# Retention in products of 64 by 64 by 64, with two state updates a chunk

## The reference, cut to what matters

```python
# q, k, v: (2 batches, 8 heads, 768 positions, 64)
gamma = 1.0 - 2.0 ** (-5.0 - np.arange(H))
for t in range(S):
    state = gamma[None, :, None, None] * state + einsum('bhd,bhe->bhde', k[:, :, t], v[:, :, t])
    y[:, :, t] = scale * einsum('bhd,bhde->bhe', q[:, :, t], state)
# x = y as (1536 tokens, 512); first mixture, 8 experts, F = 1024
P = exp(x @ w_gate - max); 8 rounds of row and column normalisation
out += P[:, e:e+1] * (maximum(x @ w1[e], 0) @ w2[e])      # for each e
# second mixture: 4 experts, weights from domain_probs, same form
```

## Time and profile before

| what | us |
|---|---|
| median of 3 runs (1549.5 to 1549.5) | 1549.5 |
| the profiled execution | 1548.59 |
| its span, first to last instruction | 1546.8 |
| PE busy | 1538.3 |
| DVE busy | 882.2 |
| ACT busy | 441.6 |
| POOL busy | 55.0 |

### The profile page before, as it was taken

How to read it: one execution, slowest core, us unless ns; L and a number is a source line. 1 busy time by engine, 2 the same in 40 slices (tenths; PEclk the granted TensorE clock), 3 DMA queues, 4 the chain that set the end, 5 groups by cost and what they waited for, 6 DMA issues and landing times.

```text
span 1546.8 us, 21387 instructions
## 1 busy us (share of the span) xinstructions
PE 1538.3 (99%) x8312; PEld 1395.1 (90%) x8312; DVE 882.2 (57%) x1419; ACT 441.6 (29%) x840; POOL 55.0 (4%) x45
## 2 busy tenths in 40 slices
PE   8999999999999999999999999999999999999999
PEld 7889988998899889988998899889998999899988
DVE  8656855555546545555464455576555556455553
ACT  4422321322223213222232132243331223213311
POOL 6200000000000000000000000012000000000000
PEclk9999999999999999999999999999999999999999
DMA  9100101101001011010010110101101001011011
GB/s 347 57 28 28 55 1 55 42 14 55 26 29 54 0 54 39 16 54 24 30 54 0 54 40 16 55 1 56 55 1 55 28 28 54 0 54 55 1 43 67
DMA packets 34602, 66.62 MB, mean 43 GB/s; under 512 B 2032, under 2 KB 2672, under 8 KB 34544
## 3 DMA queue, kind: packets, MB, share of 16 engines
q1 hardware_dynamic: 34112, 65.63, 12.2%
q10 hardware_dynamic: 432, 0.18, 0.0%
HBM read 62.66 MB, written 3.15 MB: 43 GB/s over the span
## 4 chain that ended last, share of the span: by engine, by line
PE 98%; DVE 1%; DMA 1%; issue 0%; SPq 0%; DVEq 0%
PE banks L1151 17%; PE banks L1152 17%; PE banks L1150 17%; PE banks L1129 15%; PE banks L1133 15%; PE banks L1131 15%; PE banks L1007 1%; DMA qt_in<-in_q_t 0%; PE banks L1042 0%; PE banks L1093 0%; PE banks L1037 0%; DMA small<-in_c_small 0%; DVE scores L637 0%; PE banks L1026 0%; PE banks L1073 0%; PE banks L1075 0%
## 5 line engine op out<-in xcount | busy, mean ns | idle before, releaser
L1129 PE MATMUL banks<-x_hi,w_hi 128*128 128x384 f32 x1344 | 449.9, 335 | 1.4 <-DVE w_lo L665 1.3
L1133 PE MATMUL banks<-x_hi,w_lo 128*128 128x384 f32 x1344 | 449.5, 334 | 0.0
L1131 PE MATMUL banks<-x_lo,w_hi 128*128 128x384 f32 x1344 | 449.3, 334 | 0.0
L1152 PE MATMUL banks<-w_hi,h_lo 128*128 128x512 f32 x1148 | 447.6, 390 | 0.0
L1151 PE MATMUL banks<-w_lo,h_hi 128*128 128x512 f32 x1148 | 447.4, 390 | 0.0
L1150 PE MATMUL banks<-w_hi,h_hi 128*128 128x512 f32 x1148 | 446.9, 389 | 0.0
L866 DVE SCALAR_TENSOR_TENSOR acc<-banks,gate,acc 128x512 f32<-128x512 f32 x251 | 188.5, 751 | 372.5 <-PE banks L1152 372.5
L540 ACT COPY ups<-banks 128x384 f32<-128x384 f32 x288 | 138.1, 480 | 900.5 <-PE banks L1133 900.3
L818 DVE TENSOR_TENSOR ups<-banks,ups 128x384 f32<-128x384 f32 x288 | 155.5, 555 | 190.2 <-ACT ups L540 168.4
L1129 PEld LDWEIGHTS banks<-x_hi,w_hi 128*128 128x128 f32 x1344 | 252.4, 188 | 4.0 <-DVE w_lo L665 2.0
L1152 PEld LDWEIGHTS banks<-w_hi,h_lo 128*128 128x128 f32 x1148 | 215.4, 188 | 44.9
(11 more groups left out here) (100 smaller groups left out, 492.9 us busy)
## 6 DMA issues: line engine op xcount, KB each, us to landing
w_raw<-in_moe_w SPq DMA_DIRECT2D x46, 1024.0 KB, 5.0
kt_in<-in_k_t SPq DMA_DIRECT2D x12, 256.0 KB, 4.3
qt_in<-in_q_t SPq DMA_DIRECT2D x12, 256.0 KB, 5.7
v_in<-in_v SPq DMA_DIRECT2D x12, 256.0 KB, 5.9
k_in<-in_k SPq DMA_DIRECT2D x10, 256.0 KB, 5.8
out<-acc SPq DMA_DIRECT2D x2, 768.0 KB, 3.5
out<-acc SPq DMA_DIRECT2D x5, 256.0 KB, 2.0
w_raw<-in_moe_w SPq DMA_DIRECT2D x4, 256.0 KB, 6.3
```

The costliest lines, as they stand in the source:

```text
L1129: nc.tensor.matmul(o, w1_hi[:, w, kc, fs], x_hi[:, x, kc, at], start=start and kc == 0, stop=False, skip_group_check=True)
L1131: nc.tensor.matmul(o, w1_hi[:, w, kc, fs], x_lo[:, x, kc, at], start=False, stop=False, skip_group_check=True)
L1133: last = nc.tensor.matmul(o, w1_lo[:, w, kc, fs], x_hi[:, x, kc, at], start=False, stop=kc == 1, skip_group_check=True)
L1152: last = nc.tensor.matmul(o, h_lo[:, f, b, rows], w2_hi[:, f, :], start=False, stop=(n == UC - 1))
```

## The change

The chunk stays at 128 positions for loads, but products take 64 positions, so every one is 64 by 64 by 64. Scores are made for the two diagonal halves only (16 matmuls in place of 8, half the columns and half the output rows). The state is kept for the start and for the middle of each chunk: `to_state(j)` adds the first half of step j+1 and the second half of step j, `state_out` copies both out, and `from_state` serves both halves of the chunk. `from_scores` runs in two parts: in the first, rows 0 to 63 serve heads 0 to 3 and rows 64 to 127 heads 4 to 7, in the second the other way round; the second waits for the first (`y_half`). k of the last chunk is now loaded, its first 64 positions, and decayed. `k_dec` and `q_up` have two buffers a batch. Masks and powers are 64 long; scores lie in one pair of banks; one instruction masks a step. SP waits for each tensor's own reader, three steps back. The buffer `x_raw` goes: sums of x are written where their low parts will be, in `x_lo` (the name `x_whole` is the same memory in float32), and `sums_low` of chunks 3, 4 and 5 runs on POOL behind the weight sums. The warm-up matmuls and the experts are as they were.

```diff
-DOUBLINGS = 4
-LOADED = P >> DOUBLINGS
+HP = P // 2
+DOUBLINGS = 3
+LOADED = HP >> DOUBLINGS
+GROUPS = HEADS + 2 * DC
...
+        with ExitStack() as whole:
+            x_whole = sb("x_whole", [P, 7, 2, SEQ], F32, whole)
...
-            k_dec = [sb(f"k_dec{b}", [P, HEADS, HD], F32, att) for b in range(BATCH)]
-            q_up = [sb(f"q_up{b}", [P, DC, P], F32, att) for b in range(BATCH)]
-            scores = [sb(f"scores{r}", [P, 2, DC, P], F32, att) for r in range(2)]
-            state = [sb(f"state{b}", [P, DC, HD], F32, att) for b in range(BATCH)]
-            sb("clear", [P, 512], F32, att)
+            k_dec = [[sb(f"k_dec{r}{b}", [P, HEADS, HD], F32, att) for b in range(BATCH)] for r in range(2)]
+            q_up = [[sb(f"q_up{r}{b}", [P, 2, DC, HP], F32, att) for b in range(BATCH)] for r in range(2)]
+            scores = [sb(f"scores{r}", [P, HEADS, HP], F32, att) for r in range(2)]
+            state = sb("state", [P, 2 * BATCH, DC, HD], F32, att)
...
+        ps_scores = two_banks[0].rearrange("p (r x) -> p r x", r=2)[:, :, 0:DC * HP]
+        ps_kv = two_banks[1].rearrange("p (b x) -> p b x", b=BATCH)[:, :, 0:DC * HD]
...
+        def x_sums_at(n):
+            return x_whole[:, X_T1:X_T4 + 1, :, x_at(n)]
...
+                n = P if c < CH - 1 else HP
+                sp.dma_start(k_in[r][b][0:n, :, :], k[b, c, 0:n].rearrange("t (h d) -> t h d", h=HEADS)).then_inc(
                     k_in_s[r][b], 16)
...
+                    sp.wait_ge(scored, s - 4 + 1)
+                    sp.wait_ge(q_raised, s - 4 + 1)
+                load_qk(c, b)
+                if c > 1:
+                    sp.wait_ge(k_decayed, s - 4 + 1)
+                load_k(c, b)
+                if c > 1:
                     sp.wait_ge(y_done, s - 4 + 1)
-                load_qk(c, b)
-                load_kv(c, b)
+                load_v(c, b)
                 if 5 <= s < 5 + DC:
...
             def decay_k(s):
                 c, b = s // BATCH, s % BATCH
+                n = P if c < CH - 1 else HP
                 pool.wait_ge(k_in_s[c % 2][b], 16 * (c // 2) + 16)
-                if c > 0:
-                    pool.wait_ge(kv_done, s - 1)
-                nc.gpsimd.tensor_tensor(k_dec[b][:, :, :], k_in[c % 2][b][:, :, :],
-                                        kdecay[:, c, :].unsqueeze(2).to_broadcast([P, HEADS, HD]),
+                if c > 1:
+                    pool.wait_ge(kv_done, s - 4 + 2)
+                nc.gpsimd.tensor_tensor(k_dec[c % 2][b][0:n, :, :], k_in[c % 2][b][0:n, :, :],
+                                        kdecay[0:n, c, :].unsqueeze(2).to_broadcast([n, HEADS, HD]),
                                         ALU.mult).then_inc(k_decayed, 1)
             def raise_q(s):
                 c, b = s // BATCH, s % BATCH
+                half = slice(1 if c == 0 else 0, 2)
                 pool.wait_ge(qk_in[c % 2][b], 32 * (c // 2) + 32)
-                if c == 1:
+                if c == 0:
                     pool.wait_ge(rise_made, 1)
                 else:
-                    pool.wait_ge(rise_ready, c - 1)
-                    pool.wait_ge(y_done, s - 1)
-                nc.gpsimd.tensor_tensor(q_up[b][:, :, :], qt_in[c % 2][b][:, :, :], rise[c % 2][:, :, :],
-                                        ALU.mult).then_inc(q_raised, 1)
+                    pool.wait_ge(rise_ready, c)
+                if c > 1:
+                    pool.wait_ge(y_done, s - 4 + 1)
+                nc.gpsimd.tensor_tensor(q_up[c % 2][b][:, half, :, :],
+                                        qt_in[c % 2][b].rearrange("p c (n i) -> p n c i", n=2)[:, half, :, :],
+                                        rise[c % 2][:, half, :, :], ALU.mult).then_inc(q_raised, 1)
...
+                pool.wait_ge(x_lot, n)
+                nc.gpsimd.tensor_tensor(x_lo[:, X_T1:X_T4 + 1, :, x_at(n)], x_sums_at(n),
...
-            for s in range(BATCH, STEPS - BATCH):
+            for s in range(STEPS):
+                if s == STEPS - 2:
+                    first_w1_sum(0)
+                if s == STEPS - 1:
+                    first_w1_sum(1)
                 raise_q(s)
-                decay_k(s)
-            first_w1_sum(0)
-            raise_q(STEPS - 2)
-            first_w1_sum(1)
-            raise_q(STEPS - 1)
+                if s < STEPS - 1:
+                    decay_k(s + 1)
             first_w1_sum(2)
             first_w1_sum(3)
-            sums_low(CH - 1)
+            for n in range(CPB, CH):
+                sums_low(n)
...
-            def state_out(s, b):
-                act.wait_ge(kv_done, s + 1)
-                nc.scalar.copy(state[b][:, :, :], ps_kv[:, b * DC * HD:(b + 1) * DC * HD].rearrange(
-                    "p (c e) -> p c e", c=DC)).then_inc(state_ready, 1)
+                nc.scalar.copy(x_hi[:, X_T1:X_T4 + 1, :, x_at(n)], x_sums_at(n)).then_inc(x_hit, 1)
+            def state_out(j):
+                act.wait_ge(kv_done, j + 2)
+                b = j % BATCH
+                banks = slice(0, BATCH) if 0 <= j < STEPS - BATCH else slice(1 - b, 2 - b)
+                if j < 0 or j >= STEPS - BATCH:
+                    halves = slice(2 * (1 - b) + 1, 2 * (1 - b) + 2)
+                else:
+                    halves = slice(0, 4, 3) if b == 0 else slice(1, 3)
+                nc.scalar.copy(state[:, halves, :, :], ps_kv[:, banks, :].rearrange(
+                    "p b (c e) -> p b c e", c=DC)).then_inc(state_ready, 1)
...
+            state_out(-1)
+            rise_out(1)
...
-                for r in range(2):
-                    dve.wait_ge(scored, 2 * s + r + 1)
-                    nc.vector.tensor_tensor(scores[s % 2][:, r, :, :],
-                                            score_bank(s, r).rearrange("p (c i) -> p c i", c=DC),
-                                            mask[:, r, :, :], ALU.mult).then_inc(masked, 1)
+                dve.wait_ge(scored, s + 1)
+                nc.vector.tensor_tensor(scores[s % 2].rearrange("p (r c) i -> p r (c i)", r=2), ps_scores,
+                                        powers[:, 0:HEADS, :].rearrange("p (r c) i -> p r (c i)", r=2),
+                                        ALU.mult).then_inc(masked, 1)
...
+                dve.wait_ge(x_summed, n + 1)
                 low(x_lo[:, X_B11:X_B22 + 1, :, x_at(n)], x_blocks(n), x_hi[:, X_B11:X_B22 + 1, :, x_at(n)]).then_inc(x_lob, 1)
...
-                    sums_low(c - 1)
+                    if c <= CPB:
+                        sums_low(c - 1)
+            x_sums(CH - 1)
...
             def score(s):
                 c, b = s // BATCH, s % BATCH
                 pe.wait_ge(qk_in[c % 2][b], 32 * (c // 2) + 32)
                 if s > 0:
-                    pe.wait_ge(masked, 2 * s - 1)
+                    pe.wait_ge(masked, s)
                 for i in range(DC):
                     for r in range(2):
-                        last = nc.tensor.matmul(score_bank(s, r)[:, i * P:(i + 1) * P], kt_in[c % 2][b][rows_of(DC * r), i, :],
-                                                qt_in[c % 2][b][rows_of(DC * r), i, :], start=True, stop=True)
-                        if i == DC - 1:
-                            last.then_inc(scored, 1)
-            def attend(s):
+                        for p in range(2):
+                            last = nc.tensor.matmul(ps_scores[half_rows(p), r, i * HP:(i + 1) * HP],
+                                                    kt_in[c % 2][b][rows_of(DC * r), i, half_rows(p)],
+                                                    qt_in[c % 2][b][rows_of(DC * r), i, half_rows(p)],
+                                                    start=True, stop=True)
+                last.then_inc(scored, 1)
+            def y_of(s, h, p):
                 c, b = s // BATCH, s % BATCH
-                def y(h):
-                    at = x_col(b, h // 2)
-                    return x_banks(c)[h % 2 * HD:h % 2 * HD + HD, at:at + P]
+                at = x_col(b, h // 2) + p * HP
+                return x_banks(c)[h % 2 * HD:h % 2 * HD + HD, at:at + HP]
+            def from_state(s):
+                c, b = s // BATCH, s % BATCH
                 if c > 1 and b == 0:
                     x_read(c - 2)
-                if c > 0:
-                    pe.wait_ge(state_ready, s - 1)
-                    pe.wait_ge(q_raised, s - 1)
-                    for h in [0, 1, 4, 5, 2, 3, 6, 7]:
-                        nc.tensor.matmul(y(h), state[b][rows_of(h), h % DC, :], q_up[b][rows_of(h), h % DC, :],
-                                         start=(h % DC < 2), stop=False, skip_group_check=True)
-                pe.wait_ge(v_in_s[c % 2][b], 16 * (c // 2) + 16)
-                if c < CH - 1:
-                    pe.wait_ge(k_decayed, s + 1)
-                    if s > 0:
-                        pe.wait_ge(state_ready, s)
-                    for h in [0, 4, 1, 5, 2, 6, 3, 7]:
-                        at = HD * (DC * b + h % DC)
```

(61 more changed lines are left out.)

## The result

The change makes the kernel slower: 1562.9 us (1561.1 to 1564.2, 6 runs) against 1549.3 (1548.8 to 1549.5, 6 runs). The ratio is 1.0087, interval 1.0074 to 1.0100. The forecast was 1547.9 with a range to 1551.6, so the time lies 11 us outside.

The account below looks back on a forecast made before the run. PE, 98% of the chain that ended last, was taken as the bound, so the start of product 1 of the first `up` decides: 47.3 instead of 48.95 us. Thus 1549.5 - 1.6 = 1547.9 us, range 1546.6 to 1551.6.

Parts of the forecast that it names:

- 0.058 us for four: Retention products on PE: four 64x64 pairs with 64 moving columns, running at once, cost 0.058 us.
- Value taken: 2.1 us a step for PE against 3.18: Retention step on PE: 128 pairs as 32 fours, 1.86 us, plus about 0.2 for breaks at waits.
- At 2.1 us a step PE outruns the data: Retention: transfers become late next, a step's 1.05 MB taking 2.7 us at 390 GB/s, 3.4 with a piece of w1.
- `t` = 36.3: End of retention loads: time in us when k of step 10 lands, taken between 35.9 and 37.2.
- `raise_q(11)` at 43.6: POOL's tail: last raise of q ends at t + 7.0 + 0.3 for contention, 43.6 us against 43.33 before.
- The gain of 1.6 us: Hand-over to the experts: product 1 of the first `up` starts at 47.3 instead of 48.95, 1.6 us earlier.
- Bounds: 0 to 0.5 us, taken 0: Cost of VectorE's w1 split stalling some 2.5 us beside moved sums on POOL; product 4 needs it 8 us after `up` starts.
- The pace of small products: Rival, retention on PE: a pair costs fixed time whatever its tile; 27 ns gives +2.1, 1551.6 us; chance 0.20.
- The clock rival: Rival, retention: PE idles a third, granted clock falls to 1.2 GHz, a pair takes 28 ns; +3.4, 1552.9 us; chance 0.05.
- ScalarE's ring: Rival, retention: ScalarE's work and waits take 2.9 us a step; if other waits join, no gain, 1549.5 us; chance 0.10.
- a shorter POOL: Rival, end of retention: POOL's tail is not the bound, product 1 near 45.0; -3.9, 1545.6 us; chance 0.08.
- The chance of 0.12 for slower: Whole kernel: chance of slower by more than 0.2%, 3.1 us, from 0.4 of the small-product pace rival and most of the clock's.

Follow-up runs that it names:

- e3: The changed kernel without the loads of q, k and v for chunks 2 to 5, whose steps compute on what is in the buffers: 1558.2 us, one run.
- e7: The kernel before with its old products and the rest of the change, but sums_low of chunks 3 and 4 on VectorE again: 1549.4 us, ratio 1.0004.
- e5: The changed kernel with half of each product group left out from step 4 on, so 64 pairs a step: 1554.1 us, one run.
- e4: The kernel before with its old products and chunk updates, and all the rest of the change, moved sums included: 1550.6 us, ratio 1.0012.
- e10: The changed kernel with sums_low of chunks 3 and 4 back on VectorE: 1563.8 us, ratio 1.0097.
- e6: The kernel before with 32 tiny extra float32 products a step, which makes 128 pairs a step: 1561.8 us, one run.
- e8: e7 with VectorE's first two w_lo ahead of its chunk 4 sums of x, and ScalarE's weight-sum cast ahead of sums_high(4): 1553.3 us, ratio 1.0029.

## Why the prediction was wrong

**Products: the duration was right, what it was taken for was not.** "0.058 us for four" gave 0.46 us for a group of 32; measured are 0.52 and 0.54, some 15% more, and 126 pairs from 41.08 to 43.16, 2.1 us, at full clock. The failed step is "Value taken: 2.1 us a step for PE against 3.18". It priced a step by streams and waits alone, and left out that the instructions themselves must arrive. In its place the runs show one piece of 16 KB for 126 pairs. From 14.71, the end of the first stop, to 61.30, the end of the tenth piece after it, are 4.66 us for each. A step of 128 pairs therefore costs 4.7 us, not 2.1. The 2.1 us are what PE needs once the instructions are there; the term that the sum lacks is the wait for the next piece.

**What is late next.** "At 2.1 us a step PE outruns the data" named transfers as the next bound. They were not: the DMA share fell to 0.67 in 40 to 45 us, and without most of them (e3) `up` still came at 54.91. They only made each piece 0.7 us later. The next bound was on no list of mine, neither in the sum nor among the rivals.

**It could have been bounded from the trace of before.** Its instruction packets came at 13.7, 20.8, 27.2, 34.1, 38.7 and 44.6 us, never closer than 4.6. That was no proof of a limit, as PE asked for no more, but it was the nearest row to a resource that the change uses twice as fast. Better still, each of these packets started 0.2 to 2.6 us after PE had passed the place in its stream that belongs to it, and ended 1.6 to 3.6 us after; the old steps left 6.4 us for that, the new one leaves 2.1. At 4.6 us for 126 pairs, ten pieces behind the first stop (14.7, which only the changed kernel's trace gives) end near 60.7, and the hand-over is 14 us later: nearly the measured loss. By the method of the forecast this belonged in the list as a cost bounded by its nearest row; nothing, if the fetch stays hidden as it was before, would have been the other bound.

**GpSimd and the hand-over.** The terms `t` = 36.3 and `raise_q(11)` at 43.6 could not come true, since PE was late first. e7 comes nearest, with the old products and without k of the last chunk: `up` at 46.29, product 1 at 49.68. e5 tests the chain on POOL: from decay k(10) at 41.34 to the end of `raise_q(11)` at 48.73 are 7.4 us without a break, where the forecast had 7.0 and 0.3, and PE waits for it (2.09 us). So the length of the chain was right; there it began 5 us later than at `t` = 36.3. The gain of 1.6 us is not seen anywhere.

**Edits at no cost.** "Bounds: 0 to 0.5 us, taken 0" was too low for the moved sums with the old products: 1.2 us, e4 against e7. In the changed kernel no cost of theirs is seen (e10). The forecast looked at product 4 and the last `w1` parts. But in e4 POOL began the sums at 44.41, and the `w_lo` of products 0 and 1 lay beside them, at 3.7 and 2.8 times their duration.

**Rivals.** The pace of small products (chance 0.20) had the right sign and the wrong cause. Inside a group a pair takes 0.52 / 32, 16 ns, far below its 27. The Trainium skill's floor of about 25 ns ("TensorE: Matmul & The Clock Gate", Part 1), which gave 1549.0, is not seen in these groups either. The clock rival (0.05) did happen, but as a consequence: it fell after stops of PE. Its price for a pair at half clock, 28 ns, was right: 31.55 to 32.40 is 0.85 us for 32, 27 ns. At half clock the 126 pairs of a piece take 3.7 us (30.42 to 34.10, then a stop of 1.25), so a good part of that hides in the fetch. From stop to stop it was 4.9 and 5.7 us there against 4.2 and 4.6 from 41.08 at full clock, but more data moved there too. How much of the 13.6 us the clock holds was not measured by a run of its own, but the six runs of the changed kernel bound it. Their mean granted clocks, 0.991 to 0.997, mean some 28 to 9 us at half clock, and the two at the ends took 1562.4 and 1561.1 us, with 1563.5 at 0.995 between them. So 19 us more at half clock went with 1.3 us more, and the clock holds no large part of the loss. The chances of ScalarE's ring and of a shorter POOL were never put to the test. The chance of 0.12 for slower, from which the measured sign came, was built on other mechanisms, and none of them reaches 13 us.

## What to carry to other kernels

Cutting products into smaller ones multiplies instructions, and these have a supply of their own: count them for each microsecond as one counts bytes. Here two pairs (one float32 matmul) were four instructions, and a stretch that could use up 126 pairs in 2.1 us got them every 4.7 us and stood still in between, in the middle of groups, mostly with "issue" as the releaser; one that took 4.2 us for them (e6, from 40 us on) did not stop. Stops at a fixed count of instructions, beside packets of the instruction queue, are its mark, and moving the stream by a known number of real instructions is the cheapest proof. And an instruction that moves to GpSimd is free only if VectorE has no two SBUF tensors to subtract at that time, or if PE does not wait for them.

## What the runs showed of the hardware

- Instructions reach PE in pieces of 16 KB, 256 instructions, here 126 pairs and some waits. The average interval was 3.9 us with nearly idle DMA engines (e3) and 4.7 beside loads (the changed kernel, 3.5 to 6.3 each). The first long stop came behind 220 loads.
- In the kernel before, the changed one and e3, a packet started only after PE had passed the place that belongs to it, by 0.2 to 3.7 us, and there was one packet for each place. Whether the queue could run further ahead, no run shows.
- 64 by 64 products on four tiles start every 16 ns on average over 32 pairs at full clock.
- A subtraction of two SBUF tensors on VectorE took 2.54 us instead of 0.68 (512 elements) and 3.41 instead of 1.23 (1024) while GpSimd subtracted two SBUF tensors.
- The granted clock fell to half, 1.2 GHz, after stops of 3 us inside otherwise busy stretches (15.8 us, behind the stop of 11.7 to 14.7), and in e8 at 50.8 us, within the stop of 3.88 us that ended at 51.64. In e5 it stayed at full through a first stop of 2.72 us and fell at 20.6, in the second; in e6, with no stop over 0.7 us behind 10 us in retention, it stayed at 1.00.
